# Token gathers of a routed expert kernel: two at a time, and six of them issued later

## The reference

```python
scores = where(causal, -1e9, scale * q @ k.T + min(cum_k - cum_q, 0))     # 4 batches x 8 heads x 576 tokens x 64
x = softmax(scores) @ v                                                   # -> (4, 576, 512)
e = argmax(x @ w_gate), or the expert of the token before where sigmoid(x @ w_local) >= 0.5   # 8 experts
x = p[e] * (relu(x @ w1[e]) @ w2[e])                                      # w1 512x1024, w2 1024x512 for each expert
h = relu(x @ w_in); out = (h * sigmoid(conv3(h, conv_w))) @ w_out         # 512 -> 1024 -> 512
```

## Time and profile before

| | |
|---|---|
| median of three executions | 744.62 us (742.53 to 746.62) |
| profiled execution, its span | 744.3 us, 742.6 us |
| TensorE matmul busy | 720.5 us, 97% of the span |
| VectorE, ScalarE, GpSimd busy | 458.7, 316.1, 328.4 us |
| granted TensorE clock, mean | 0.988 of full speed |
| chain that ended last | TensorE 67% of the span |
| DMA | 115.35 MB; of it 11.28 MB on GpSimd's queue |

### The profile page before, as it was taken

How to read it: one execution, slowest core, us unless ns; L and a number is a source line. 1 busy time by engine, 2 the same in 40 slices (tenths; PEclk the granted TensorE clock), 3 DMA queues, 4 the chain that set the end, 5 groups by cost and what they waited for, 6 DMA issues and landing times.

```text
span 742.6 us, 13519 instructions
## 1 busy us (share of the span) xinstructions
PE 720.5 (97%) x4227; PEld 591.8 (80%) x4227; DVE 458.7 (62%) x1088; ACT 316.1 (43%) x634; POOL 328.4 (44%) x442
## 2 busy tenths in 40 slices
PE   8999999999979599999999999999999999999998
PEld 6676767767678487888888888888899889889986
DVE  5777778778766355566575665666399445536610
ACT  5777878778430022221412223020488335436620
POOL 8759888898236334644637647240521100000000
PEclk9999999999999799999999999999999999999999
DMA  8988888784075548786768877641421110000011
GB/s 177 217 213 227 207 224 229 210 206 134 17 216 159 137 164 273 252 271 232 256 210 300 255 241 254 220 138 44 142 64 30 43 36 15 30 30 14 29 43 56
DMA packets 114966, 115.35 MB, mean 155 GB/s; under 512 B 63804, under 2 KB 84052, under 8 KB 114900
## 3 DMA queue, kind: packets, MB, share of 16 engines
q1 hardware_dynamic: 94372, 68.54, 32.5%
q10 hardware_dynamic: 17056, 34.69, 14.2%
q0 software_dynamic: 3472, 11.28, 5.6%
HBM read 87.14 MB, written 27.34 MB: 154 GB/s over the span
## 4 chain that ended last, share of the span: by engine, by line
PE 67%; DVE 2%; another core or an unknown queue 2%; issue 1%; DMA 1%; ACT 0%; DVEq 0%; POOLq 0%; ACTq 0%
PE wide_bank L1365 18%; PE wide_bank L1694 14%; PE row_bank L1733 13%; PE row_bank L1382 9%; PE bank L1382 9%; PE bank L1331 1%; PE bank L1663 1%; DMA x_slots<-x_rows,token_of 1%; PE wide_bank L1404 0%; PE bank L1683 0%; PE wide_bank L28 0%; PE bank L1340 0%; PE row_bank L1683 0%; DVE y_sb L1524 0%
## 5 line engine op out<-in xcount | busy, mean ns | idle before, releaser
L914 POOL TENSOR_TENSOR ring<-raw_w,ring 128x2048 fp32r<-128x2048 f32 x28 | 128.7, 4619 | 117.2 <-ACT ring L904 117.2
L904 ACT ACTIVATE ring<-raw_w 128x2048 fp32r<-128x2048 f32 x30 | 55.8, 1908 | 209.3 <-DMA raw_w<-in_moe_w_dram 174.7
L1694 PE MATMUL wide_bank<-x_tr,ring 128*128 128x288 f32 x768 | 107.7, 297 | 0.0
L1694 PEld LDWEIGHTS wide_bank<-x_tr,ring 128*128 128x128 f32 x768 | 103.2, 188 | 0.9
L1733 PE MATMUL row_bank<-ring,g_tr 128*128 128x512 f32 x432 | 100.2, 390 | 0.0
L690 ACT ACTIVATE prob<-score,row_min 128x128 f32<-128x128 f32 (+2 forms) x144 | 83.4, 580 | 38.5 <-PE turn_ps L362 25.6
L1733 PEld LDWEIGHTS row_bank<-ring,g_tr 128*128 128x128 f32 x432 | 80.4, 188 | 16.2
L1785 DVE SCALAR_TENSOR_TENSOR conv<-h_pad,conv_col,conv 128x576 f32<-128x576 f32 x64 | 52.3, 817 | 53.8 <-ACT conv L1846 52.5
L252 POOL TENSOR_SCALAR bias<-ncum_row,cum_col 128x128 f32<-128x128 f32 (+3 forms) x128 | 66.8, 532 | 36.4 <-DVE row_min L551 33.4
L551 DVE CUSTOM_DVE_ANT_0 score<-score_ps,bias 128x128 f32<-128x128 f32 (+2 forms) x144 | 69.2, 514 | 19.9 <-issue 13.6
L1365 PE MATMUL wide_bank<-ring,xs_tr 128*128 x312 | 78.0, 406 | 3.3 <-DVE xs_tr L1456 1.8
(11 more groups left out here) (254 smaller groups left out, 1127.7 us busy)
## 6 DMA issues: line engine op xcount, KB each, us to landing
raw_w<-in_moe_w_dram ACTq DMA_DIRECT2D x12, 2048.0 KB, 11.2
x_slots<-h_turn SPq DMA_DIRECT2D x84, 128.0 KB, 2.9
ncum_row<-cum_rows SPq DMA_DIRECT2D x15, 512.0 KB, 4.9
y_sorted<-y_sb SPq DMA_DIRECT2D x26, 256.0 KB, 3.0
raw_w<-in_moe_w_dram SPq DMA_DIRECT2D x12, 512.0 KB, 4.4
h_turn<-h_sb SPq DMA_DIRECT2D x11, 512.0 KB, 5.3
h_turn<-x_slots SPq DMA_DIRECT2D x10, 512.0 KB, 7.2
ncum_tail<-cum_rows SPq DMA_DIRECT2D x32, 144.0 KB, 4.4
```

Source lines behind the costliest of these rows:

```text
L904: nc.scalar.activation(high, whole, ACT.Copy).then_inc(high_ready, 1)
L914: nc.gpsimd.tensor_tensor(low, whole, high.bitcast(F32), ALU.subtract).then_inc(low_ready, 1)
L1694: last = nc.tensor.matmul(wide_bank[j % 2][:, half, 0:HALF], ring[:, 0, w, col:col + P], x2_tr[:, x, kb, at:at + HALF], start=kb == 0 and ...
```

## The change

At most two gathers are on their way: gather s waits for gather s - 2. Gathers 8 to 18 stay where they were, 19 and 20 go behind `low_parts(pool, 2, 0)`, 21 and 22 behind `low_parts(pool, 3, 0)`, 23 and 24 behind `low_parts(pool, 2, 1)`. Nothing else differs; there are still 25 gathers.

```diff
     GATHERS = 4
+    IN_FLIGHT = 2
...
         for s in range(begin, end):
-            above(pool, slot_loaded[s % GATHERS], 16 * (s // GATHERS))
+            earlier = s - IN_FLIGHT
+            if earlier >= 0:
+                pool.wait_ge(slot_loaded[earlier % GATHERS], 16 * (earlier // GATHERS + 1))
             pool.indirect_dma_start(out=x_slots[:, s, :], out_offset=None, in_=x_rows,
...
-        gather_slots(pool, 8, SLOTS)
+        ahead = SLOTS - E + 2
+        gather_slots(pool, 8, ahead)
         low_parts(pool, 2, 0)
+        gather_slots(pool, ahead, ahead + 2)
         for e in range(2, E):
             low_parts(pool, e + 1, 0)
+            if e == 2:
+                gather_slots(pool, ahead + 2, ahead + 4)
             low_parts(pool, e, 1)
+            if e == 2:
+                gather_slots(pool, ahead + 4, SLOTS)
         low_parts(pool, E, 1)
```

## The result

Measured in one set of alternating executions, six of each: the changed kernel 735.47 us in the median (732.53 to 736.31), the kernel before 746.81 us (742.53 to 747.82); ratio 0.9845, 95% interval 0.9816 to 0.9874. The forecast, 733.3 against 744.62, is a ratio of 0.9848. The profiled execution of the changed kernel took 735.26 us, its span is 733.5 us, 9.1 less than before; the medians lie 11.3 apart.

What follows compares the result with a forecast made beforehand. Bound by TensorE, 97% busy, with one hole where its signals come late under three or more gathers. Gain 11.3 us, pace and moved gathers 0: 744.3 to 733.0 profiled, median 733.3 us, range 730.4 to 740.5.

Steps and rivals of the forecast that it cites:

- the wait at relu(1): Sign of being right: VectorE's 10.60 us of idling before relu(1)'s second half (L1496) gone or below 1 us.
- the pace: Gathers held to two on their way go out one per 2.1 us (1.25 to 2.8), no cost; 1.3 us kept for range.
- the full clock: Sign of being right: full granted clock from 226 us to the end of the gathers.
- hidden(2): Sign of being right: hidden matmuls of slot 2 start at 244 to 245 us instead of 254.03.
- slot 6: Sign of being right: TensorE's 24 matmuls of slot 6 at about 280.6 us; before, at 291.92.
- a hole beside one of the pairs: Sign of being wrong: a hole beside one of the three pairs of moved gathers (slots 19 to 24).
- The standstill: TensorE's signals after hidden(1) become punctual, so hidden(2) ends at 249.8 instead of 261.13 us: 11.3 us gained.
- what I had booked at 0 and kept for the range: Slot 0's late signal at the head (-1.2 us) and half clock there (1.7 us): booked 0, range down to 730.4.
- VectorE's low parts: Gathers 5 to 7 issue beside L1530; three slow issues of 2.87 us cost 5.8 of a 6.6 us margin: nothing booked.
- The pairs: Six gathers moved beside weight loads: pairs one and two together take 5.6 of 6.7 us of slack, no cost.
- The reason: Three or more gathers on their way make TensorE's signals late; with two they are punctual. Forecast's chance 0.73.
- Rival B: Another cause makes the signals late, gathers only accompany it: no gain, 744.6 us within 2 us; chance 0.12.

Runs made afterwards that it cites:

- last_pair_later: Changed kernel with only its third pair (slots 23, 24) moved behind the low parts of w1 of expert 4: 734.69 us, 1.0052 of the kernel before.
- moved_later: Changed kernel with the six gathers placed between low parts of w1 of experts 4, 5, 6 and w2 of the expert before: 731.26 us, ratio 0.9773 to kernel before.
- two_in_place: Kernel before with at most two gathers on their way, none of the six moved: 741.17 us, ratio 0.9888 to the kernel before.
- later placing: Changed kernel with the six gathers between the low parts of experts 4 to 6; in set 4 731.66 us, ratio 1.0000 to the kernel before.
- set 4: Runs on chip 1: kernel before 730.90 us, changed kernel 734.86 (1.0044), the same with its six gathers later 731.66 (1.0000).
- three_moved: Changed kernel with up to three gathers on their way instead of two, six moved: 738.99 us, ratio 0.9875 to the kernel before.
- four_moved: Changed kernel with up to four gathers on their way instead of two, six moved: 744.35 us, ratio 0.9940 to the kernel before.
- set 1: Runs on chip 10, kernel before 748.36 us: two_in_place, four_moved, three_moved and moved_later.
- two_head_only: Changed kernel with the limit of two only for slots 0 to 7, four from slot 8 on: 733.91 us, ratio 1.0046 to the kernel before.
- two_from_eight: Changed kernel with four on their way for slots 0 to 7, limit of two from slot 8 on: 735.17 us, ratio 1.0061 to the kernel before.
- set 2: Runs on chip 3, kernel before 730.48 us: changed kernel again 734.29 (1.0043), last_pair_later, two_head_only and two_from_eight.
- sets 0, 1 and 3: Set 0 is the main result (kernel before 746.81 us); in the other two the kernel before took 748.36 and 748.30 us.
- set 3: Runs on chip 3, kernel before 748.30 us: the kernel before again 748.45 (0.9997), changed kernel with its six gathers later 730.66 (0.9742).
- before_again: Kernel before, unchanged, profiled once more in set 3: 748.45 us, ratio 0.9997 to the kernel before.
- after: Profile of the changed kernel from the main result; that execution took 735.26 us.
- moved_later_third: moved_later's kernel run again in set 4, beside the changed kernel: 731.66 us, ratio 1.0000 to the kernel before.

## Why the prediction was right, and where it was not

The time came out inside the range: a ratio of 0.9845 for 0.9848, 735.47 us for 733.3 against a kernel before that itself measured 2.2 us higher in the set. That the ratios agree so closely is in part luck: the sum of the prediction was made for the profiled execution, and there the span shrank by 9.1 us and not by 11.3. Of its signs, the wait at relu(1), the pace and the full clock came as told; hidden(2) at 241.57 and slot 6 at 278.10 were earlier than the 244 to 245 and 280.6 given, and one of the signs of being wrong, a hole beside one of the pairs, appeared. By its steps:

**The standstill.** Forecast: 9.9 us of hole and 1.4 of half clock, 11.3 together. Measured: both gone, hidden(2) 13.8 us earlier, 14.7 if the later start of the gathers is counted. That the signal itself was late, and not VectorE slow to act on it, the trace of the kernel before shows directly, for it records when a semaphore was raised: `h_done`, due at 234.86 and 237.58, at 238.37 and 249.72, and `y_done`, due at 243.03, at 252.71. Nor was VectorE waiting for instructions to be loaded: the queues that carry them moved one packet at 233.90 us and the next at 260.57. The surplus of 3.4 us is for the most part what I had booked at 0 and kept for the range. Slot 0's signal is punctual: in the chain the 1.77 us have become 0.42, and the first 12 matmuls, 4.60 us before, take 3.01 at full clock. The clock part is not reliable: last_pair_later and moved_later, with the same limit, have 4.60 and 4.54 us there.

**The pace.** Forecast 2.1 us a gather, measured 1.85 in the steady part, nothing lost. The 4.19 us behind the forecast were called those of a gather alone, up to its use; they end at its landing, and three more were issued meanwhile. Two gathers, not three, fell beside VectorE's low parts (L1530, now L1539), with 2.34 and 1.90 us to issue instead of 2.87; they cost nothing, as booked. Not booked was that the load of expert 2's w1 takes longer beside gathers (see two_in_place): of the slack of 4.7 us 2.0 were left.

**The pairs.** This is the term that was mis-sized. "Both together are 5.6 of 6.7 us: no cost", and "SP's queue only carries the h_turn transfers beside them": I counted the weights' slack, for which the forecast holds (no wait of TensorE for low parts), and passed over the third thing in SP's queue, the store of the outputs, on which VectorE's next copy waits. Output(5) and output(6) cost 2.67 us of hole, 1.44 behind it and 0.4 at output(6), 4.5 in all. The later placing took 3.2 us off the changed kernel in set 4, so most of this hangs on where the pairs stand. The two misses, 3.4 us gained and 4.5 lost, nearly cancelled; the time was right partly by that.

**The reason.** Right in its place and its remedy, wrong as a rule. That three on the way make signals late by several us is refuted by three_moved. That four do is shown by four_moved in set 1 and refuted by two_head_only and two_from_eight in set 2. Rival B had the objection that the two signals of hidden(1) came 11 us apart, which depth does not explain. It was worth more than its 0.12, and a forecast for "the kernel" should have had two values, one for each condition. The changed kernel ran in three sets, and in two of them the sign is the other one: 1.0043 and 1.0044.

By the Trainium skill, "SBUF — State Buffer", "Who interferes with whom", TensorE never waits on anyone. The traces agree for most of its matmuls: the 24 of hidden(1) take 5.71 us under the deep burst of the kernel before and in the changed kernel alike. They do not agree for all: besides the two matmuls of four_moved above (0.64 and 1.00 us), TensorE stood idle inside turn_h(1) of the kernel before with no wait to be found,

```profile
244.77 0.38 PE L1404 MATMUL wide_bank<-identity,h_sb 128*128 128x128 f32 x2 [1.52 <-issue]
```

and its signals are another matter altogether in the sets 0, 1 and 3: that of hidden(1) came 12.1 us late with the deep burst of the kernel before, 0.04 with the shallow one of the changed kernel.

**What stays open.** What differs between the sets. A chip that gave one condition in set 2 gave the other in set 3, and within a set all 6 to 30 executions of the kernel before agree, so it holds for a set. Whether it is the core that was given, the place of the buffers in memory or something else that ran on the chip cannot be read from these profiles, and was not tried. Nor is the way shown by which gathers hold TensorE's signals back; that a burst of four is needed for a delay of several us, and that something else is needed too, is all that is shown. One rival was left out altogether. Under the late condition steps of landings are missing in the trace, so the recording itself may be what makes signals late. Every execution here, the timed ones too, comes with a recorded span and clock; none without recording was run.

## What to carry to other kernels

A wait without a releaser beside a punctual TensorE may be a late signal: compare the end of the instruction that raises it with the time at which the semaphore was raised, or with the start of the one that waits, before looking for a missing transfer. When DMAs are moved to another place, list everything in the queues beside them, the stores behind which a buffer comes free too, and not only what the change is about. And time a result in several sets before calling its sign known: here the same change was 1.6% faster in one and 0.4% slower in two others.

## What the runs showed of the hardware

TensorE's signals arrived 12.1 us (before) and 14.5 us (before_again) after the end of their matmuls while up to four gathers were on their way, and VectorE idled for 10.6 and 12.7 us of it. With at most three they were about 1 us late in three_moved; with at most two, signals at the first gather were 0.5 to 1.8 us late (after, two_in_place) and that of hidden(1) was acted on after 0.04 (after). All this was seen in the sets 0, 1 and 3 alone. In the sets 2 and 4 none of TensorE's signals between 212 and 262 us was late, not even with four gathers on their way, and the sets 2 and 3 ran on the same chip. The first gather had landed 4.0 to 4.2 us after its issue; with two on the way one went out per 1.85 us (after). A store of 256 KB was waited for until 9.2 us after its issue beside a weight load of 2 MB and gathers (after), and until 9.8 us after it beside a weight load without gathers (moved_later_third).
